# Expert products in chunks of 512 tokens, second product with the relu tiles stationary, state rows as a chunk of their own

## The chip, the cores and the metric

One core of one Trainium2 chip runs the whole program. The metric is the device time of one execution in microseconds (us), lower is better; the times are medians over repeated executions. TensorE multiplies, VectorE (DVE), ScalarE (ACT) and GpSimd (POOL) work on what it leaves in PSUM and SBUF, and SyncE (SP) issues the DMAs.

## What is computed

The reference takes x (4 batches, 8 heads, 512 tokens, 64 wide) and 32 state rows for each batch and head. Attention between tokens and state rows in both directions gives 4 x 544 = 2176 rows of 512 numbers, 512 token rows and 32 state rows for each batch. Then come a dense MLP and eight gated experts:

```python
h = x @ w_in                      # 512 -> 2048
x = (h - np.tanh(h)) @ w_out      # 2048 -> 512
logits = x @ w_gate               # 8 columns
P = np.exp(logits - logits.max())
for _ in range(8):                # Sinkhorn: rows, then columns
    P /= P.sum(1, keepdims=True) + 1e-09
    P /= P.sum(0, keepdims=True) + 1e-09
    P *= N / E
for e in range(E):                # w1: 512 -> 1024, w2: 1024 -> 512
    out += P[:, e:e + 1] * (np.maximum(x @ w1[e], 0.0) @ w2[e])
```

## The kernel before

**Precision.** Most products are made of three: an operand is split into a high part of type fp32r and the rest (w1h and w1l, xh and xl, w2h and w2l, hh and hl), and high x high, high x low and low x high are summed in PSUM. ScalarE makes the high parts and VectorE or GpSimd the low ones. One logical 128-deep product is therefore three matmuls, each with a weight load of its own.

**Stages.** Attention is first (lines 700 to 739 and 961 to 1015 belong to it and to what follows from it). The dense MLP goes over four half blocks of 512 hidden features (`dense`, DH = 4 passes), in each first over the 128 state rows (plain f32 operands, lines 1048 and 1079, 128 columns) and then over four batches of 512 token columns (lines 1059 to 1061 and 1075 to 1077). Its sums stand in `acc`, with features in the partitions and the 2176 rows as columns.

**Experts.** Eight experts follow. Each goes over C = 5 chunks of columns, four of 436 and one of 432 (`N`, `width`, `cols`). A chunk has eight steps f. `up` (lines 1106 to 1108) makes one tile of 128 hidden features: 4 slices k of the input x 3 parts = 12 matmuls, with the w1 tile stationary and the chunk's columns of xh or xl moving. ScalarE then writes the relu, rounded, to hh (line 579), and VectorE the rest to hl (line 782). Two steps later `down` (lines 1120 to 1122) adds this tile's share to four PSUM banks `ypsum`, one for each 128 output features: 12 matmuls, with slices of w2h and w2l stationary and hh or hl moving. There are three hidden tiles, and three PSUM banks for them (NH).

**Gates.** In the first expert's first chunk TensorE makes the logits (lines 1144 and 1145). ScalarE copies them out, SP stores them to DRAM, and loads them back with rows in the partitions (`lg_two`). VectorE and GpSimd run the Sinkhorn steps in chunk 2, and SP stores the gates and loads each expert's row of them, spread to all partitions (`gate`, 218 KB for a chunk). The first expert's outputs are kept in `acc` (line 886) and multiplied by GpSimd later (line 458). For each further chunk VectorE multiplies the four banks by the gate into `ytmp` (line 900), GpSimd adds this to `acc` (line 465), and when all four are done the banks are given free (`s_yfree`). At the end the last two adds are VectorE's (line 944), and SP stores the output by chunks.

**Weights.** During an expert's last chunk ScalarE and VectorE split the next expert's weights (lines 480, 484, 690, 694), and SP loads the tiles behind them.

## Time and profile before

| | |
|---|---|
| median of 3 runs | 1907.54 us (1907.45 to 1908.94) |
| profiled execution, first to last instruction | 1907.4 us |
| TensorE matmul busy | 1888.4 us, 99% of the span |
| TensorE weight load busy | 1744.5 us, 91% |
| VectorE busy | 632.2 us, 33% |
| ScalarE busy | 412.6 us, 22% |
| GpSimd busy | 240.4 us, 13% |
| DMA moved | 64.70 MB |

The profile has no time for the profiled execution beside its span; the median of the runs is 0.1 us above the span. PE is the matmul row of TensorE and PEld its weight loads, which overlap the matmuls. Matmuls are pipelined: the time given for one is from its start to its modelled end, and the next has started by then. So what a matmul costs is the distance from its start to the next one's start, which the text calls its pitch. Lines are those of the kernel printed above.

### The profile page before, as it was taken

Reading aid. Unit: us, or ns where it says so; the run is one execution under the profiler, and the core shown is the slowest. Engines: PE = TensorE matmul, PEld = TensorE weight load, DVE = VectorE, ACT = ScalarE, POOL = GpSimd, SP = SyncE. Lnnn points to the kernel's source line nnn. Section 1 sums busy time; section 2 is a strip of 40 time slices with the busy share of each in tenths; the row PEclk is TensorE's granted clock in tenths of the full one; section 3 lists DMA queues with packets and bytes.
Section 4 is the critical chain, followed back from the end, with each engine's and each line's share of the span. In section 5 each row is a group of like instructions: output and inputs, shape, how many; then the busy total and the mean of one; then the engine's idle time right before and its main releaser. Section 6 shows DMA issues by size and latency. Waiting matters only on the chain.

```text
span 1907.4 us, 24434 instructions
## 1 busy us (share of the span) xinstructions
PE 1888.4 (99%) x9480; PEld 1744.5 (91%) x9480; DVE 632.2 (33%) x1067; ACT 412.6 (22%) x781; POOL 240.4 (13%) x216
## 2 busy tenths in 40 slices
PE   7999999999999999999999999999999999999998
PEld 5887888899999999999999999999999999999998
DVE  6656566533333113311321132113211421142112
ACT  6434444421121112111211121112111211121110
POOL 5100000320312000200110011001100110020001
PEclk9899999999999999999999999999999999999999
DMA  6100101110121002000200020002000200010001
GB/s 226 45 17 27 44 0 50 45 46 1 39 69 34 5 5 77 26 5 5 76 26 5 5 76 26 5 5 76 26 5 5 78 24 5 5 49 24 19 19 37
DMA packets 38700, 64.70 MB, mean 34 GB/s; under 512 B 8896, under 2 KB 16656, under 8 KB 38160
## 3 DMA queue, kind: packets, MB, share of 16 engines
q1 hardware_dynamic: 38672, 64.34, 11.1%
q8 instruction: 16, 0.26, 0.1%
q14 instruction: 12, 0.10, 0.0%
HBM read 59.66 MB, written 4.67 MB: 34 GB/s over the span
## 4 chain that ended last, share of the span: by engine, by line
PE 97%; DVE 1%; ACT 1%; issue 0%; DMA 0%; POOL 0%; DVEq 0%; SPq 0%; ACTq 0%; POOLq 0%
PE bank L1108 13%; PE bank L1106 13%; PE bank L1120 13%; PE bank L1121 13%; PE bank L1107 13%; PE bank L1122 13%; PE bank L1075 3%; PE bank L1077 3%; PE bank L1076 3%; PE bank L1061 1%; PE bank L1060 1%; PE bank L1059 1%; PE bank L1015 1%; PE bank L1048 1%; PE bank L1002 1%
## 5 line engine op out<-in xcount | busy, mean ns | idle before, releaser
L782 DVE SCALAR_TENSOR_TENSOR hl<-bank,hh 128x436 fp32r<-128x436 f32 (+1 forms) x320 | 195.5, 611 | 965.1 <-ACT hh L579 964.9
L1108 PE MATMUL bank<-xh,w1l 128*128 (+2 forms) x1280 | 460.7, 360 | 0.0
L1120 PE MATMUL bank<-hh,w2h 128*128 128x436 f32 (+1 forms) x1280 | 460.6, 360 | 0.0
L1121 PE MATMUL bank<-hl,w2h 128*128 128x436 f32 (+1 forms) x1280 | 460.1, 359 | 0.0
L1106 PE MATMUL bank<-xh,w1h 128*128 (+2 forms) x1280 | 460.1, 359 | 0.0
L1122 PE MATMUL bank<-hh,w2l 128*128 128x436 f32 (+1 forms) x1280 | 459.7, 359 | 0.0
L1107 PE MATMUL bank<-xl,w1h 128*128 (+2 forms) x1280 | 459.1, 359 | 0.0
L579 ACT ACTIVATE hh<-bank 128x436 fp32r<-128x436 f32 (+1 forms) x320 | 170.9, 534 | 1233.0 <-PE bank L1108 1233.0
L465 POOL TENSOR_TENSOR acc<-acc,ytmp 128x436 f32<-128x436 f32 (+1 forms) x138 | 156.7, 1169 | 1164.9 <-DVE ytmp L900 1164.9
L1107 PEld LDWEIGHTS bank<-xl,w1h 128*128 128x128 f32 x1280 | 240.6, 188 | 13.3
L1122 PEld LDWEIGHTS bank<-hh,w2l 128*128 128x128 f32 x1280 | 240.3, 188 | 12.6
L1108 PEld LDWEIGHTS bank<-xh,w1l 128*128 128x128 f32 x1280 | 240.3, 188 | 12.4
L1121 PEld LDWEIGHTS bank<-hl,w2h 128*128 128x128 f32 x1280 | 240.6, 188 | 12.0
L1106 PEld LDWEIGHTS bank<-xh,w1h 128*128 128x128 f32 x1280 | 240.3, 188 | 12.3
L1120 PEld LDWEIGHTS bank<-hh,w2h 128*128 128x128 f32 x1280 | 240.3, 188 | 11.5
L900 DVE TENSOR_TENSOR ytmp<-bank,gate 128x436 f32<-128x436 f32 (+1 forms) x140 | 84.0, 611 | 143.0 <-PE bank L1122 138.2
L1075 PE MATMUL bank<-hh,w2h 128*128 128x512 f32 x256 | 101.8, 398 | 0.0
L1077 PE MATMUL bank<-hh,w2l 128*128 128x512 f32 x256 | 101.4, 396 | 0.0
L1076 PE MATMUL bank<-hl,w2h 128*128 128x512 f32 x256 | 101.4, 396 | 0.0
L777 DVE TENSOR_TENSOR hl<-h_less_tanh,hh 128x512 fp32r<-128x512 f32 x64 | 45.3, 708 | 44.0 <-ACT hh L574 44.0
L1075 PEld LDWEIGHTS bank<-hh,w2h 128*128 128x128 f32 x256 | 48.1, 188 | 12.7 <-DVE acc L795 1.1
L1077 PEld LDWEIGHTS bank<-hh,w2l 128*128 128x128 f32 x256 | 48.2, 188 | 11.7
(101 smaller groups left out, 1166.5 us busy)
## 6 DMA issues: line engine op xcount, KB each, us to landing
st<-w SPq DMA_DIRECT2D x160, 256.0 KB, 2.7
gate<-gate_scratch SPq DMA_DIRECT2D x32, 218.0 KB, 3.0
xT<-xT SPq DMA_DIRECT2D x8, 512.0 KB, 8.2
xn<-xn SPq DMA_DIRECT2D x4, 1024.0 KB, 6.2
out<-acc SPq DMA_DIRECT2D x4, 872.0 KB, 4.2
gate<-gate_scratch SPq DMA_DIRECT2D x8, 216.0 KB, 3.1
out<-acc SPq DMA_DIRECT2D x2, 432.0 KB, 2.8
sT<-sT SPq DMA_DIRECT2D x2, 128.0 KB, 3.8
```

The lines of the kernel that those rows point to most:

```text
L465: nc.gpsimd.tensor_tensor(acc[:, k, cols(c)], acc[:, k, cols(c)], ytmp[:, k % 3, 0:width(c)], ALU.add).then_inc(s_ya, 1)
L579: nc.scalar.activation(hh[:, f % NH, 0:n], hpsum[f % NH][:, 0:n], ACT.Relu).then_inc(s_hh, 1)
L782: v.scalar_tensor_tensor(hl[:, f % NH, 0:n], hpsum[f % NH][:, 0:n], 0.0, hh[:, f % NH, 0:n].bitcast(f32), ALU.max, ALU.subtract).then_inc( ...
L1075: mm(out, w2h[:, s, at], high, start=(s == 0), stop=False)
L1076: mm(out, w2h[:, s, at], hl[:, i % NH, :], start=False, stop=False)
L1077: last = mm(out, w2l[:, s, at], high, start=False, stop=(s == HF - 1))
L1106: mm(out, w1h[:, f, k, :], xh[:, k, cols(c)], start=(k == 0), stop=False)
L1107: mm(out, w1h[:, f, k, :], xl[:, k, cols(c)], start=False, stop=False)
L1108: last = mm(out, w1l[:, f, k, :], xh[:, k, cols(c)], start=False, stop=(k == KT - 1))
L1120: mm(out, w2h[:, f, at], hh[:, f % NH, 0:n], start=(f == 0), stop=False)
L1121: mm(out, w2h[:, f, at], hl[:, f % NH, 0:n], start=False, stop=False)
L1122: last = mm(out, w2l[:, f, at], hh[:, f % NH, 0:n], start=False, stop=(f == F - 1))
```

## The change

- The 2048 token rows and the 128 state rows are kept apart: xh and xl hold the token columns alone (`own_rows`), and new tiles `xsh`, `xsl` the state rows.
- An expert has C = 4 chunks of 512 tokens and, after chunk 1 (`ST_CHUNK`), one of the 128 state rows (`state_up`, `state_down`).
- `down` is turned round: a slice of 128 tokens of hh or hl is stationary, and 512 columns of w2h or w2l move. The outputs have tokens in the partitions (`yacc`, 17 tiles of 128 x 512).
- The gate of a token is then one number for each partition. VectorE multiplies and adds in one instruction (`scalar_tensor_tensor` in `gated`), and gives each bank free alone. GpSimd's adds, the gate tiles, their DMAs and the DRAM scratch go. VectorE copies an expert's gates to a small tile first (`own_gate`), and multiplies the first expert's kept outputs in chunk 3 (`gate_kept`).
- The logits are turned by 17 transposes on TensorE (`turn_logits`) in place of the way through DRAM.
- The output is stored by tokens, the last chunk in four parts of one tile each. Loops over chunks are written out on TensorE and ScalarE.

```diff
-C = 5
-N = 436
+C = B
+ST_TILE = TQ - 1
+ST_CHUNK = 1
+PASSES = C + 1
...
             def up(b, c, f):
...
-                out = hpsum[f % NH][:, 0:width(c)]
+                out = hpsum[f % NH][:]
                 for k in range(KT):
-                    mm(out, w1h[:, f, k, :], xh[:, k, cols(c)], start=(k == 0), stop=False)
-                    mm(out, w1h[:, f, k, :], xl[:, k, cols(c)], start=False, stop=False)
-                    last = mm(out, w1l[:, f, k, :], xh[:, k, cols(c)], start=False, stop=(k == KT - 1))
+                    mm(out, w1h[:, f, k, :], xh[:, k, own_rows(c)], start=(k == 0), stop=False)
+                    mm(out, w1h[:, f, k, :], xl[:, k, own_rows(c)], start=False, stop=False)
+                    last = mm(out, w1l[:, f, k, :], xh[:, k, own_rows(c)], start=False, stop=(k == KT - 1))
                 last.then_inc(s_up, 1)
...
-                if f == 0:
-                    pe.wait_ge(s_yfree, q + 1)
-                for k in range(KT):
-                    out, at = ypsum[k][:, 0:n], slice(k * P, (k + 1) * P)
-                    mm(out, w2h[:, f, at], hh[:, f % NH, 0:n], start=(f == 0), stop=False)
-                    mm(out, w2h[:, f, at], hl[:, f % NH, 0:n], start=False, stop=False)
-                    last = mm(out, w2l[:, f, at], hh[:, f % NH, 0:n], start=False, stop=(f == F - 1))
+                for t in range(ST):
+                    if f == 0:
+                        pe.wait_ge(s_yfree, ST * q + t + 1)
+                    out, at = ypsum[t][:], slice(t * P, (t + 1) * P)
+                    mm(out, hh[:, f % NH, at], w2h[:, f], start=(f == 0), stop=False)
+                    mm(out, hh[:, f % NH, at], w2l[:, f], start=False, stop=False)
+                    last = mm(out, hl[:, f % NH, at], w2h[:, f], start=False, stop=(f == F - 1))
...
+            def state_up(f):
+
+                out = hpsum[f % NH][:, 0:SB]
+                for k in range(KT):
+                    mm(out, w1h[:, f, k, :], xsh[:, k, :], start=(k == 0), stop=False)
+                    mm(out, w1h[:, f, k, :], xsl[:, k, :], start=False, stop=False)
+                    last = mm(out, w1l[:, f, k, :], xsh[:, k, :], start=False, stop=(k == KT - 1))
+                last.then_inc(s_up, 1)
+
+            def state_down(x, f):
+
+                pe.wait_ge(s_hs, DSTEPS + turn(x, C) * F + f + 1)
+                if f == 0 and (not isinstance(x, int) or x):
+                    pe.wait_ge(s_syf, x)
+                mm(stpsum[:], hh[:, f % NH, 0:SB], w2h[:, f], start=(f == 0), stop=False)
+                mm(stpsum[:], hh[:, f % NH, 0:SB], w2l[:, f], start=False, stop=False)
+                last = mm(stpsum[:], hl[:, f % NH, 0:SB], w2h[:, f], start=False, stop=(f == F - 1))
+                if f == F - 1:
+                    last.then_inc(s_sy, 1)
+
+            def state_rows(x):
+
+                for f in range(F):
+                    state_up(f)
+                    if f >= 2:
+                        state_down(x, f - 2)
+                state_down(x, F - 2)
+                state_down(x, F - 1)
...
+            def turn_logits():
+
+                pe.wait_ge(s_lgc, C + 1)
+                for t in range(TQ):
+                    last = nc.tensor.transpose(lgpsum[:, t * 2 * E:(t + 1) * 2 * E], lg_rows[:, t * P:(t + 1) * P],
+                                               ident[0:2 * E, 0:2 * E])
+                last.then_inc(s_lgt, 1)
...
+            def state_input():
+
+                for k in range(KT):
+                    act.wait_ge(s_dsum, KT * (1 + (DH - 1) * DC) + k + 1)
+                    nc.scalar.copy(by_batch(xsh, k), states(acc, k)).then_inc(s_x2h, 1)
...
             def gated(x, c):
...
-                    v.tensor_tensor(ytmp[:, k % 3, 0:n], ypsum[k][:, 0:n], gate[:, c, 0:n], ALU.mult).then_inc(s_ym, 1)
-                dve.wait_ge(s_ym, (x - 1) * (C * KT) + (c + 1) * KT)
-                dve.sem_inc(s_yfree, 1)
+                for t in range(ST):
+                    i = c * ST + t
+                    dve.wait_ge(s_y, ST * (x * C + c) + t + 1)
+                    v.scalar_tensor_tensor(yacc[:, i], ypsum[t][:], gcur[:, i:i + 1], yacc[:, i], ALU.mult,
+                                           ALU.add).then_inc(s_yfree, 1)
...
+            store(ST, 0, ST)
+            store(2 * ST, ST, 2 * ST)
+            sp.wait_ge(s_syf, E)
+            sp.dma_start(out_d[:, ST_TILE:TQ], yacc[:, ST_TILE:TQ]).then_inc(s_out, 16)
+            store(3 * ST, 2 * ST, 3 * ST)
+            for t in range(3 * ST, 4 * ST):
+                store(t + 1, t, t + 1)
```

## Rows read from the trace of the kernel before

**Rows 1.** The page: busy time by engine, and the chain's shares.

```profile
PE 1888.4 (99%) x9480; PEld 1744.5 (91%) x9480; DVE 632.2 (33%) x1067; ACT 412.6 (22%) x781; POOL 240.4 (13%) x216
PE 97%; DVE 1%; ACT 1%; issue 0%; DMA 0%; POOL 0%; DVEq 0%; SPq 0%; ACTq 0%; POOLq 0%
```

**Rows 2.** Busy time by windows, the expert stage and one inner stretch of it.

```profile
core 0: us, PE busy (x) PEld busy (x) DVE busy (x) ACT busy (x) POOL busy (x), PEclk, DMA share, GB/s
377.45:1901.52 1524.07, 1524.07 (x7720) 1449.74 (x7719) 395.88 (x668) 239.05 (x453) 192.03 (x174) 1.00 0.09 28
422.00:612.00 190.00, 190.00 (x965) 180.72 (x964) 65.36 (x145) 29.98 (x57) 27.39 (x30) 1.00 0.12 35
```

**Rows 3.** Timeline of TensorE, the expert stage's first and last matmuls.

```profile
377.22 0.39 PE L1077 MATMUL bank<-hh,w2l 128*128 128x512 f32 x1
377.45 0.36 PE L1106 MATMUL bank<-xh,w1h 128*128 128x436 f32 x1
...
1901.52 0.35 PE L1122 MATMUL bank<-hh,w2l 128*128 128x432 f32 x1
```

**Rows 4.** Timeline of TensorE, a dense stretch of 512 columns, 66 matmuls from first to last.

```profile
80.18 0.40 PE L1075 MATMUL bank<-hh,w2h 128*128 128x512 f32 x1
...
82.98 0.40 PE L1059 MATMUL bank<-xh 128*128 128x512 f32 x1
...
95.57 0.39 PE L1059 MATMUL bank<-xh 128*128 128x512 f32 x1
```

**Rows 5.** The chain: 16 plain f32 passes of 64 columns, then 24 of 128.

```profile
22.27 1.73 PE bank L1002 x16
...
299.40 2.68 PE bank L1048 x24
```

**Rows 6.** Weight loads, groups by line and shape.

```profile
L1106 PEld LDWEIGHTS bank<-xh,w1h 128*128 128x128 f32 x1280 | 240.3, 188 | 12.3
L1002 PEld LDWEIGHTS bank<-a2T,xn 128*128 128x128 f32 x128 | 16.8, 209 | 0.9 <-issue 0.5
L1079 PEld LDWEIGHTS bank<-state_tokens_hidden,st 128*128 128x128 f32 x128 | 16.2, 191 | 0.7
```

**Rows 7.** VectorE and ScalarE groups by line and shape.

```profile
L795 DVE TENSOR_TENSOR acc<-bank,acc 128x512 f32<-128x512 f32 x64 | 40.8, 684 | 11.4 <-PE bank L1077 11.3
L769 DVE TENSOR_TENSOR state_tokens_hidden<-bank,tanh_h 128x128 f32<-128x128 f32 x16 | 4.6, 286 | 3.4 <-ACT tanh_h L564 3.4
L564 ACT ACTIVATE tanh_h<-bank 128x128 f32<-128x128 f32 x16 | 4.4, 278 | 26.3 <-PE bank L1048 24.5 <-DVE state_tokens_hidden L769 1.0
L694 DVE TENSOR_TENSOR w2l<-st,w2h 128x512 fp32r<-128x512 f32 x63 | 57.2, 925 | 0.9
L777 DVE TENSOR_TENSOR hl<-h_less_tanh,hh 128x512 fp32r<-128x512 f32 x64 | 45.3, 708 | 44.0 <-ACT hh L574 44.0
```

**Rows 8.** Timeline of VectorE at the end.

```profile
1900.27 2.44 DVE L900 TENSOR_TENSOR ytmp<-bank,gate 128x432 f32<-128x432 f32 x4 [4.15 <-PE bank L1122]
1902.86 1.25 DVE L944 TENSOR_TENSOR acc<-acc,ytmp 128x432 f32<-128x432 f32 x2
```

**Rows 9.** DMA issues: size of one, median us from issue to landing.

```profile
st<-w SPq DMA_DIRECT2D x160, 256.0 KB, 2.7
gate<-gate_scratch SPq DMA_DIRECT2D x32, 218.0 KB, 3.0
out<-acc SPq DMA_DIRECT2D x2, 432.0 KB, 2.8
```

More of the change, by code:

```diff
@@ L112, in build @@
         amax = sb("amax", [P, 1])
-        assert place[0] <= gates + C * N * 4
+        hiddens = place[0]
+        hh = sb("hh", [P, NH, S], f32r)
+        hl = sb("hl", [P, NH, S], f32r)
+        xsh = sb("state_rows_hi", [P, KT, SB], f32r)
+        xsl = sb("state_rows_lo", [P, KT, SB], f32r)
+        scratch = place[0]
+        end = place[0]
+        place[0] = scratch
+        wg_raw = sb("wg_raw", [P, KT, E])
+        wg = sb("wg", [P, KT, P], f32r)
+        lg_rows = sb("lg_rows", [2 * E, T])
+        lg_two = sb("lg_two", [P, TQ, 2 * E])
+        end = max(end, place[0])
         place[0] = after_w2l - (F - HF) * DM * 4
@@ L146, in build @@
         r1 = sb("r1", [P, 2, 4 * ST])
-        end = max(end, place[0])
+        assert place[0] <= scratch
         assert end <= nc.sbuf_usable_end, (end, nc.sbuf_usable_end)
@@ L156, in build @@
         lgpsum = bank[7]
+        stpsum = bank[7]
         mpsum = bank[7]
@@ L529, in m_hi @@
                     rows = slice(pair_first(b, kp), pair_first(b, kp) + 2 * NS)
-                    nc.scalar.copy(xh[rows, 2 + kp // 2, batch(b)], bank[rows, :]).then_inc(s_mh, 1)
+                    nc.scalar.copy(xh[rows, 2 + kp // 2, own_rows(b)], bank[rows, :]).then_inc(s_mh, 1)
             for i in range(2):
@@ L598, in dense @@
                         w1_hi(DENSE, HF + s)
+                    if last and s == 2 and j == 1:
+                        state_input()
                     if last and s == 2 and j >= 2:
@@ L614, in logits_exp, with chunk @@
                     nc.scalar.activation(pr[:], pr[:], ACT.Exp, bias=amax[:, 0:1]).then_inc(s_exp, 1)
-            def chunk(b, c, split, extra=None):
-                q = (b - DENSE) * C + c
+            def chunk(b, c, extra=None):
+                x, q = b - DENSE, (b - DENSE) * C + c
+                split = c == C - 1 and extra is not last_chunk
                 for f in range(F):
-                    hidden_expert(q, f, width(c))
+                    hidden_expert(turn(x, c), f)
                     if extra is not None:
@@ L865, in sinkhorn, with chunk @@
                 rows(f)
-            def chunk(b, c, split, extra=None):
-                q = (b - DENSE) * C + c
+            def chunk(b, c, extra=None):
+                x, q = b - DENSE, (b - DENSE) * C + c
+                split = c == C - 1 and extra is not last_chunk
                 for f in range(F):
-                    hidden_expert(q, f, width(c))
+                    hidden_expert(turn(x, c), f)
                     if extra is not None:
@@ new lines, in _, with gate_some @@
+            chunk(DENSE, 0, gating)
+            dve.wait_ge(s_x2s, (C + 1) * KT)
+            keep(0)
+            chunk(DENSE, 1, logits_max)
+            keep(1)
+            state_rows(0)
+            keep_states()
+            chunk(DENSE, 2, sinkhorn)
+            keep(2)
+            columns(SINKHORN - 1)
+            def gate_some(f):
+                for t in range(2 * f, min(2 * f + 2, 3 * ST)):
+                    gate_kept(t)
+                if f == F - 1:
+                    gate_kept(ST_TILE)
@@ L930, in _, with expert @@
+            chunk(DENSE, 3, gate_some)
+            gated_first(3)
             last_w2(DENSE)
-            def expert(b, split):
+            def expert(b, end=False):
+                x = b - DENSE
+                own_gate(x)
                 for c in range(C):
-                    chunk(b, c, split and c == C - 1)
-                    gated(b - DENSE, c)
-                if split:
-                    last_w2(b)
-            with dve.Fori(DENSE + 1, NB - 1) as b:
-                expert(b, True)
@@ L941, in _ @@
-            expert(NB - 1, False)
-            for k in range(KT // 2, KT):
-                v.tensor_tensor(acc[:, k, cols(C - 1)], acc[:, k, cols(C - 1)], ytmp[:, k % 3, 0:width(C - 1)],
-                                ALU.add).then_inc(s_last, 1)
+                    chunk(b, c, last_chunk if end else None)
+                    gated(x, c)
+                    if c == ST_CHUNK:
+                        state_rows(x)
+                        gated_states(x)
+                if not end:
+                    last_w2(b)
@@ L1153, in _ @@
             dense(DH - 1, last=True)
-            pe.wait_ge(s_x2s, KT)
+            pe.wait_ge(s_x2s, 2 * KT)
             chunk(DENSE, 0, gating=True)
-            with pe.Fori(1, C - 1) as c:
+            pe.wait_ge(s_lgr, 1)
+            for c in range(1, C):
                 chunk(DENSE, c)
-            chunk(DENSE, C - 1)
             with pe.Fori(DENSE + 1, NB) as b:
-                with pe.Fori(0, C - 1) as c:
+                for c in range(C):
                     chunk(b, c)
-                chunk(b, C - 1)
 def kernel(**inputs):
```

304 lines of the change are left out of this document (131 added, 173 removed).

## The prediction

> **What bounds the kernel now.** I read the busy times and the chain's shares first [rows 1]: TensorE's matmuls are busy for 99% of the span, and 97% of the chain that ended last is TensorE. No other engine passes 33%. Busy time alone says little where matmuls overlap, so I next asked the windows for the expert stage from its first matmul to its last [rows 2], whose ends come from TensorE's timeline [rows 3]: 1524.07 us, 7720 matmuls, granted clock 1.00 (2.4 GHz). TensorE is busy through every one of these microseconds. 7720 is 8 experts x 5 chunks x 8 steps x 24 = 7680, and 40 for the logits. The mean pitch is 1524.07 / 7720 = 197.4 ns. The inner stretch gives 190.00 / 965 = 196.9 ns, so there is no place where the stage stalls. The chunks' mean width is 2176 / 5 = 435.2 columns, so a column costs 197.4 / 435.2 = 0.4536 ns.
>
> So the expert stage is a gapless stream of matmuls, and what VectorE, GpSimd and SP do beside it costs nothing as long as it stays beside it. The change is worth what it does to the number of matmuls and their pitch, plus what it does behind the last matmul.
>
> **Matmuls removed and added.** The columns that move are the same. Up: 12 matmuls over 2176 columns in each step, before and after. Down, before: 12 over 2176 columns = 26112. Down, after: 12 of 512 columns for each of four chunks and 3 for the states, 51 x 512 = 26112. What changes is how they are cut:
> - 512 columns: up 12 x 4 x 64 = 3072, down 3072, state down 3 x 64 = 192, logits 4 x 8 = 32. Together 6368.
> - 128 columns, each with a weight load of 128 columns: state up 12 x 64 = 768, logits 8. Together 776.
> - 17 transposes of logits, 16 columns each.
>
> Together 7161 in place of 7720.
>
> **Price at 512 columns.** The dense stage has the same kind (three-part products, a load for each, the same clock). From 80.18 to 95.57 us there are 66 of them, 12 down and 6 up in turn, without a gap [rows 4]: 15.39 / 66 = 233.2 ns. The per-column price of the expert stage gives 0.4536 x 512 = 232.3 ns. I take 232.5. Turning the down product round puts a hidden tile in the load and w2 in the stream; both sides of the dense products (1059 to 1061 have xh on both sides, 1075 to 1077 hidden tiles moving) run at nearly the same pitch, 2.80 us for 12 from 80.18 to 82.98 (233.3), so I give the turning itself nothing. Low end: if the excess over the bare column time, 197.4 - 435.2 / 2.4 = 16.1 ns, is one fixed price for each matmul, 512 columns cost 213.3 + 16.1 = 229.4. High end 234.
>
> 6368 x 232.5 = 1480.6 us.
>
> **Price at 128 columns.** No row before shows an fp32r matmul under 432 columns, and on this one unknown most of the result hangs. Lowest bound: the column price alone, 0.4536 x 128 = 58 ns; with the fixed 16.1 it is 53.3 + 16.1 = 69.4. Nearest rows in size: the plain f32 passes, of which two make one product. 24 of 128 columns take 2.68 us, 111.7 ns each; 16 of 64 columns take 1.73 us, 108 ns each [rows 5]. Half the columns save almost nothing, so at these sizes something other than the columns sets the pitch, and each of these passes has its load of 128 columns. The loads of fp32r take 188 ns by the record and those of plain f32 191 [rows 6], start to end with the latency in it, so I expect the same floor for both kinds. At 436 or 512 columns the load is hidden behind the stream; behind 128 columns it isn't. Highest bound: a whole product at 128 columns costs no less in this mode than in plain f32, two passes, 2 x 111.7 = 223.4 ns. I take 111.7, since the rows say "load", and loads of both kinds look alike.
>
> 776 x 111.7 = 86.7 us. 17 transposes at 111.7 (loads again) = 1.9 us.
>
> The Trainium skill (TensorE: Matmul & The Clock Gate, section LDWEIGHTS) puts a load at the columns of the stationary operand over 1.2 GHz, 106.7 ns for 128. The trace agrees with it at the small sizes, 108 and 111.7 [rows 5]; by 106.7 the two terms above would be 4 us less. The same page's section on the back-to-back gap gives N / 2.4 + 2.5 ns for a matmul alone, 184 at 436 columns against the measured 197.4, and some 81 ns for pairs of load and matmul at 128 columns; by 81 the state rows would cost 24 us less than I count.
>
> **Sum of the stage.** 1480.6 + 86.7 + 1.9 = 1569.2 us against 1524.07: +45.1 us. Put as a balance: the 6368 at 232.5 and the transposes leave (1524.1 - 1482.5) / 776 = 53.6 ns for each 128-column matmul before the change loses, and the columns alone take 53.3.
>
> **What lies beside it, and costs nothing.** VectorE in a chunk of 48 x 4 = 192 matmuls, 44.6 us: eight hl tiles at about 0.7 us (L777) and four gated tiles at 0.68 (L795, [rows 7], the same operands of one bank and one of SBUF) are 8.4 us; with sixteen splits at up to 0.93 in the last chunk 23 us. `gate_kept` adds 13 x 0.7 us in one chunk. All of that is cover of over 20 us a chunk. If it were gone the 4 x 0.68 us would stand in front of the next chunk's `down`. It has three `up` tiles, 36 x 0.2325 = 8.4 us, before it needs a bank, and the banks come free one at a time. GpSimd's multiplies and adds go, and free time that nobody waits for. The gate DMAs (218 KB each, [rows 9]) go from SP's queue; behind them there stood only the weight loads, whose consumers have a whole chunk.
>
> State rows: a step is 12 x 0.112 + 3 x 0.2325 = 2.0 us of TensorE against one relu of 128 columns, 0.28 us, and one rest, 0.29 us [rows 7]. At the end `state_down(7)` needs its hidden tile 1.4 us after the last `state_up`, and relu and rest take about 0.65 with their hand-overs. At 58 or 70 ns a step is 1.4 us or more, still covered. At the start VectorE has the fourth bank to gate (0.7 us) before the first state tile; TensorE has three `state_up`, 4.0 us. `turn_logits` waits for a copy whose logits TensorE made a step (5.6 us) earlier. `state_input` is four small ScalarE copies (about 0.28 each) in the last dense pass, over a step of some 4.9 us. The Sinkhorn steps get 5.6 us for each f instead of 4.7. `own_gate` is one small copy on VectorE behind the last bank. I price all these waits at 0 to 3 us together and take 0.
>
> **The end.** Before: last matmul starts at 1901.52 and ends near 1901.9, VectorE's last multiply ends at 1902.71, its two adds at 1904.11 [rows 8], then 3.3 us to the end of the span for issue, landing (2.8, [rows 9]) and waiting. After: one fused instruction of 0.68 us from about 1901.95, then a DMA of 256 KB, 2.7 in place of 2.8 (st<-w). End to end 0.68 + 3.2 instead of 5.5: -1.5 us.
>
> **Total** 1907.4 + 45.1 - 1.5 = 1951.0 us, 2.3% slower. This is against the profiled span, which is 0.1 us under the median; I predict 1951. Its own range: 512 columns at 229.4 to 234 is -20 to +10 us, waits 0 to +3, so 1931 to 1964.
>
> **Rivals.**
> - *Narrow matmuls are charged as full f32.* If fp32r at 128 columns loses its single pass and costs what two plain passes do, 223.4 ns, the 776 cost 173.4 us: 1951.0 + 86.7 = 2037.7. For it: no narrow fp32r matmul is in the trace, and the kernel's narrow products (L1048, L1079) are of the plain kind. Against it: nothing but the similar loads. Chance 0.27.
> - *The load hides, the fixed price stays.* 776 x 69.4 = 53.9, so 1480.6 + 53.9 + 1.9 = 1536.4, +12.3 - 1.5: 1918.2. The 108 ns at 64 columns speaks against it, unless plain f32 loads are slower than they look. Chance 0.08.
> - *Columns alone.* All matmuls cost 0.4536 ns a column. The columns are equal, so only transposes and the end are left: 1907.4 + 1.9 - 1.5 = 1907.8, no change. Chance 0.06.
> - *Faster: fewer matmuls, each with a fixed price.* With 229.4 at 512 and 69.4 at 128 columns: 1460.8 + 53.9 + 1.9 = 1516.6, -7.5 - 1.5: 1898.4. It decides once 512 columns cost 229.4 and a 128-column matmul stays under (1524.1 + 1.5 - 1460.8 - 1.9) / 776 = 81 ns. For it: 559 matmuls less, and 16.1 ns of excess on each. Against it: 233.2 measured at 512 columns and 108 at 64. Chance 0.09.
>
> The skill's isolated gap is the page's form of the last two: by it the stage would come out the same, since 6368 at 215.8 and 776 at 55.8 equal 7720 at about 184. The trace has 197.4 and 233.2 in those places.
>
> **How the numbers follow.** The forecast has 0.50, the rivals 0.27, 0.08, 0.06 and 0.09. What a measurement of this kernel can tell from no change is about 0.2%, 3.8 us. Slower: 0.50 + 0.27 + 0.08 = 0.85. Same 0.06, faster 0.09. The range must hold the forecast's own 1931 to 1964 and the first rival's 2038, since leaving out the latter alone would lose 0.27; it reaches down to 1918 for the second. 1915 to 2042.
>
> **What would show it.** In the profile after, the stream of 512-column matmuls should have a pitch of 232 to 233 ns in up and in turned down alike. The twelve matmuls of `state_up` should follow each other at 112 ns: 8 experts x 96 x 112 ns is the 86 us. Their pitch is the number that decides between all cases (58, 69, 112, 223). TensorE should have no gap over 0.3 us at the edges of chunks and of state rows. The expert stage should begin near 377.5 us, and about 4.0 us should lie between the last matmul's end and the end of the span. The forecast is wrong if the state pitch is far from 112, if 512 columns cost another price with the hidden tiles stationary (6368 matmuls: each ns is 6.4 us), or if the written-out loops or the state rows' hand-overs make TensorE stop.

## The result and the profile after

The changed kernel takes 1943.46 us (median, 1942.33 to 1944.25), the kernel before 1908.24 us beside it (1907.45 to 1909.29). The ratio is 1.0182, with a 95% interval of 1.017 to 1.0194: 35 us slower.

The profiled execution of after spans 1940.2 us, and its own time is 1942.33, so 2.1 us lie around the span. For the kernel before that distance is 1.8 us wherever a span and a time of the same execution are known (1908.86 against 1907.1, 1907.53 against 1905.7): its profiled span of 1907.4 belongs to an execution of about 1909.2 us, and the 0.1 us that stands ahead of the prediction compares different executions. So the spans differ by 32.8 us and the medians by 35.2. Busy time by engine, the chain's shares, and the queue that brings instructions, from the page of after (they answer to [rows 1]):

```profile
PE 1920.1 (99%) x8921; PEld 1576.4 (81%) x8921; DVE 626.7 (32%) x1061; ACT 413.6 (21%) x782; POOL 59.8 (3%) x58
q8 instruction: 77, 1.26, 0.3%
PE 97%; issue 1%; DVE 1%; ACT 1%; POOL 0%; DVEq 0%; ACTq 0%; POOLq 0%
```

TensorE has 559 matmuls less and is busy 32 us longer. GpSimd fell from 240 to 60 us, and nobody waited for that. The windows of the expert stage, whose ends come from TensorE's timeline (they answer to [rows 2, 3]):

```profile
378.94:1936.52 1557.58, 1557.58 (x7161) 1284.28 (x7160) 390.28 (x664) 238.40 (x450) 9.20 (x13) 1.00 0.07 22
```

```profile
378.70 0.40 PE L1081 MATMUL bank<-hh,w2l 128*128 128x512 f32 x1
378.94 0.40 PE L1110 MATMUL bank<-xh,w1h 128*128 128x512 f32 x1
...
1936.52 0.39 PE L1126 MATMUL bank<-w2h,hl 128*128 128x512 f32 x1
```

The stage went from 1524.07 to 1557.58 us, +33.5, at the same clock and still busy from end to end. The rest of the difference lies at the two ends of the span: the stage starts 1.49 us later (378.94 against 377.45), and between the last matmul's start and the end of the span there are 3.7 us where there were 5.9, -2.2. Sum: 33.5 + 1.5 - 2.2 = 32.8 us, the difference of the spans (1940.2 - 1907.4).

Three kinds of matmul are to be seen in TensorE's timeline. Inside one step, twelve up matmuls (the last three are shown), then twelve down (the first is shown), and the next step's first up:

```profile
600.75 0.39 PE L1110 MATMUL bank<-xh,w1h 128*128 128x512 f32 x1
600.97 0.39 PE L1111 MATMUL bank<-xl,w1h 128*128 128x512 f32 x1
601.20 0.39 PE L1112 MATMUL bank<-xh,w1l 128*128 128x512 f32 x1
601.43 0.39 PE L1124 MATMUL bank<-w2h,hh 128*128 128x512 f32 x1
...
604.24 0.40 PE L1110 MATMUL bank<-xh,w1h 128*128 128x512 f32 x1
```

The ups shown follow each other at about 0.227 us; the twelve downs take 604.24 - 601.43 = 2.81, 234 ns each. And at the start of the state rows, 36 `state_up` matmuls:

```profile
477.05 0.40 PE L1126 MATMUL bank<-w2h,hl 128*128 128x512 f32 x1
477.28 0.22 PE L1134 MATMUL bank<-state_rows_hi,w1h 128*128 128x128 f32 x1
477.34 0.27 PE L1135 MATMUL bank<-state_rows_lo,w1h 128*128 128x128 f32 x1
477.45 0.27 PE L1136 MATMUL bank<-state_rows_hi,w1l 128*128 128x128 f32 x1
...
481.13 0.28 PE L1136 MATMUL bank<-state_rows_hi,w1l 128*128 128x128 f32 x1
481.25 0.45 PE L1144 MATMUL bank<-w2h,hh 128*128 128x512 f32 x1
```

From 477.34 to 481.25 there are 35 pitches, 111.7 ns each. The first narrow one has a pitch of only 0.06: its load ran behind the wide matmul before it. The bill comes on the other side, where a wide one (L1144) follows on narrow ones.

Summing all distances between starts over the stage gives the whole account:

| kind | number | predicted each, sum | measured mean, sum |
|---|---|---|---|
| up, 512 columns | 3072 | 232.5 ns, 714.2 us | 227.5 ns, 699.0 us |
| down turned, 512 | 3072 | 232.5, 714.2 | 234.1, 719.1 |
| state down, 512 | 192 | 232.5, 44.6 | 244.5, 46.9 |
| state up, 128 | 768 | 111.7, 85.8 | 108.2, 83.1 |
| logits, 512 and 128 | 40 | 8.3 us | 8.3 us |
| transposes | 17 | 111.7, 1.9 | 68.6, 1.2 |
| together | 7161 | 1569.2 us | 1557.6 us |

What lies beside the stream, from the groups by line and shape, VectorE's timeline at the end, and the DMA issues (they answer to [rows 6 to 9]):

```profile
L1134 PEld LDWEIGHTS bank<-state_rows_hi,w1h 128*128 128x128 f32 x256 | 49.0, 191 | 2.1
L747 DVE SCALAR_TENSOR_TENSOR hl<-bank,hh 128x512 fp32r<-128x512 f32 x256 | 177.2, 692 | 909.1 <-ACT hh L532 909.1
L881 DVE SCALAR_TENSOR_TENSOR yacc<-bank,gate_now,yacc 128x512 f32<-128x512 f32 x112 | 80.1, 751 | 132.8 <-PE bank L1126 132.8
```

```profile
1934.85 2.85 DVE L881 SCALAR_TENSOR_TENSOR yacc<-bank,gate_now,yacc 128x512 f32<-128x512 f32 x4 [5.00 <-PE bank L1126]
```

```profile
out<-yacc SPq DMA_DIRECT2D x5, 256.0 KB, 2.0
```

The fused gate and add takes 751 ns, and VectorE waits for TensorE before it, not the other way round. The last of the four ends at 1937.70, and 2.5 us later the span ends.

### The profile page after: what moved, and what is told of

Same layout as the page of the kernel before. It is cut to its first block, busy times and chain, and to the rows that moved or that the text cites. A ratio compares the mean times of both kernels' runs of the same rounds, so it can differ in the third digit from the quotient of the medians.

```text
span 1940.2 us, 22124 instructions
## 1 busy us (share of the span) xinstructions
PE 1920.1 (99%) x8921; PEld 1576.4 (81%) x8921; DVE 626.7 (32%) x1061; ACT 413.6 (21%) x782; POOL 59.8 (3%) x58
## 3 DMA queue, kind: packets, MB, share of 16 engines
q8 instruction: 77, 1.26, 0.3%
## 4 chain that ended last, share of the span: by engine, by line
PE 97%; issue 1%; DVE 1%; ACT 1%; POOL 0%; DVEq 0%; ACTq 0%; POOLq 0%
PE bank L1124 12%; PE bank L1126 12%; PE bank L1125 12%; PE bank L1110 12%; PE bank L1112 12%; PE bank L1111 12%; PE bank L1079 3%; PE bank L1081 3%; PE bank L1080 3%; PE bank L1136 1%; PE bank L1135 1%; PE bank L1063 1%; PE bank L1064 1%; PE bank L1065 1%; PE bank L1134 1%; PE bank L1019 1%
## 5 line engine op out<-in xcount | busy, mean ns | idle before, releaser
L747 DVE SCALAR_TENSOR_TENSOR hl<-bank,hh 128x512 fp32r<-128x512 f32 (+1 forms) x320 | 195.8, 612 | 1002.2 <-ACT hh L532 1002.2
L1124 PE MATMUL bank<-w2h,hh 128*128 128x512 f32 x1024 | 406.9, 397 | 0.0
L1126 PE MATMUL bank<-w2h,hl 128*128 128x512 f32 x1024 | 405.5, 396 | 0.0
L1125 PE MATMUL bank<-w2l,hh 128*128 128x512 f32 x1024 | 404.9, 395 | 0.0
L1110 PE MATMUL bank<-xh,w1h 128*128 128x512 f32 x1024 | 399.8, 390 | 0.0
L1111 PE MATMUL bank<-xl,w1h 128*128 128x512 f32 x1024 | 399.0, 390 | 0.0
L1112 PE MATMUL bank<-xh,w1l 128*128 128x512 f32 x1024 | 398.9, 390 | 0.0
L1126 PEld LDWEIGHTS bank<-w2h,hl 128*128 128x128 f32 x1024 | 193.1, 189 | 47.8
L1125 PEld LDWEIGHTS bank<-w2l,hh 128*128 128x128 f32 x1024 | 192.5, 188 | 46.5
L1124 PEld LDWEIGHTS bank<-w2h,hh 128*128 128x128 f32 x1024 | 192.2, 188 | 44.2
```

The source lines that it names most:

```text
L747: v.scalar_tensor_tensor(hl[:, f % NH, 0:n], hpsum[f % NH][:, 0:n], 0.0, hh[:, f % NH, 0:n].bitcast(f32), ALU.max, ALU.subtract).then_inc( ...
L1110: mm(out, w1h[:, f, k, :], xh[:, k, own_rows(c)], start=(k == 0), stop=False)
L1111: mm(out, w1h[:, f, k, :], xl[:, k, own_rows(c)], start=False, stop=False)
L1112: last = mm(out, w1l[:, f, k, :], xh[:, k, own_rows(c)], start=False, stop=(k == KT - 1))
L1124: mm(out, hh[:, f % NH, at], w2h[:, f], start=(f == 0), stop=False)
L1125: mm(out, hh[:, f % NH, at], w2l[:, f], start=False, stop=False)
```

## The experiments

Times of timed kernels are medians, with a ratio to the kernel before on the same chip. "One run" is one profiled execution, read for its pitches and not for its time.

### Narrow matmuls of other sizes (one run)

The sizes of `state_up` go by its steps f: two as in the change, two with 64 moving columns, two with 256 (token columns), two with 64 columns of w1 stationary. Its output isn't the reference's.

```diff
             def state_up(f):
...
+                    elif f < 4:
+                        out = bank_f[:, 0:64]
+                        mm(out, w1h[:, f, k, :], xsh[:, k, 0:64], start=first, stop=False)
...
+                    elif f < 6:
+                        out = bank_f[:, 0:256]
+                        mm(out, w1h[:, f, k, :], xh[:, k, 0:256], start=first, stop=False)
...
+                    else:
+                        out = bank_f[0:64, 0:SB]
+                        mm(out, w1h[:, f, k, 0:64], xsh[:, k, :], start=first, stop=False)
```

> The changed kernel, with the state rows' first product cut four ways by step, so its numbers are not the reference's: steps 0 and 1 as they are (128 columns move, 128 are stationary), 2 and 3 with 64 moving, 4 and 5 with 256 moving, 6 and 7 with 128 moving and only 64 stationary. Theory (the weight load sets the pitch of a narrow matmul): 112 ns, then 108 to 112 at 64 moving (no gain), about 120 at 256 moving (256 / 2.4 = 107 and the 14 of the 512-column stream), and 59 to 70 with 64 stationary columns. Rival (a narrow fp32r matmul runs at two cycles a column, 128 x 2 / 2.4 = 107 ns): about 58 at 64 moving, 213 or more at 256 moving unless that counts as wide, and 112 unchanged with 64 stationary.

TensorE's timeline of this kernel: 64 columns moving, 256 moving, and 128 moving behind a stationary tile of 64 columns:

```profile
484.25 0.28 PE L1144 MATMUL bank<-state_rows_hi,w1l 128*128 128x64 f32 x1
484.36 0.28 PE L1142 MATMUL bank<-state_rows_hi,w1h 128*128 128x64 f32 x1
...
486.05 0.28 PE L1149 MATMUL bank<-xh,w1l 128*128 128x256 f32 x1
486.16 0.28 PE L1147 MATMUL bank<-xh,w1h 128*128 128x256 f32 x1
486.28 0.28 PE L1148 MATMUL bank<-xl,w1h 128*128 128x256 f32 x1
...
490.23 0.22 PE L1152 MATMUL bank<-state_rows_hi,w1h 128*64 128x128 f32 x1
490.29 0.22 PE L1153 MATMUL bank<-state_rows_lo,w1h 128*64 128x128 f32 x1
```

Medians over the eight experts, by line: 111 to 112 ns for 128 moving columns, 111 to 112 for 64, 117.5 to 120 for 256, and 59 to 60 for 128 columns behind a load of 64. So at 128 moving columns and fewer neither the columns nor a fixed price sets the pitch, the load does, and it goes with the columns of the stationary tile. The loads' own records agree: 192 ns for 128 stationary columns and 135 for 64. The Trainium skill (TensorE: Matmul & The Clock Gate, section LDWEIGHTS) has a load at its columns over 1.2 GHz, 106.7 ns for 128 and 53.3 for 64; the runs show 112 and 60, a few ns more.

### Narrow matmuls mixed in among wide ones (4 runs)

All the computation stays; in chunk 1 each down matmul is followed by one narrow matmul that is extra work, into the bank of the state rows before these use it.

```diff
                     mm(out, hh[:, f % NH, at], w2h[:, f], start=(f == 0), stop=False)
+                    if c == ST_CHUNK:
+                        mm(stpsum[:, 0:SB], w1h[:, f, t, :], xsh[:, t, :], start=True, stop=True)
```

(and the same behind the other two parts, with xsl and w1l)

> The changed kernel with 96 more narrow matmuls for each expert, 768 in all (copies of the state rows' first product whose result is overwritten), one behind each wide matmul of chunk 1's second product. Theory (each narrow matmul exposes the load of the next one, wherever it stands): +112 ns each, +86 us, 2029 us. Rival (behind a wide matmul two loads fit, so a narrow one costs its columns alone, 58 to 60 ns): +45 us, 1988 us; then mixing the state rows into the token chunks would give back some 40 us.

2027.66 us, ratio 1.0623 (1.0607 to 1.0639). Over the changed kernel that is 84.2 us for 768 extra matmuls, 110 ns each. TensorE's timeline:

```profile
1258.62 0.39 PE L1124 MATMUL bank<-w2h,hh 128*128 128x512 f32 x1
1258.85 0.22 PE L1126 MATMUL bank<-state_rows_hi,w1h 128*128 128x128 f32 x1
1258.91 0.44 PE L1127 MATMUL bank<-w2l,hh 128*128 128x512 f32 x1
1259.19 0.22 PE L1129 MATMUL bank<-state_rows_lo,w1h 128*128 128x128 f32 x1
1259.25 0.45 PE L1130 MATMUL bank<-w2h,hl 128*128 128x512 f32 x1
```

A narrow one has a pitch of 0.06 and the wide one behind it 0.28, together 340 ns, where a wide one alone has 234. As I read it, the narrow one hides its own load behind the wide one, but the next load has only the narrow one's 128 columns to hide behind. So placing narrow matmuls between wide ones gives nothing back. What helps is not to have them.

### No chunk of its own for the state rows (11 runs)

The whole computation, with the turned down product. The 17 tiles of 128 rows, state rows as the last, go in five chunks of 3, 3, 4, 4 and 3 tiles, so up moves 384 or 512 columns and never 128.

```diff
-ST_CHUNK = 1
-PASSES = C + 1
+CHUNKS = ((0, 3), (3, 3), (6, 4), (10, 4), (14, 3))
+NC = len(CHUNKS)
...
-        xh = sb("xh", [P, KT, B * S], f32r)
+        xh = sb("xh", [P, KT, T], f32r)
```

> The whole computation. The second product stays turned, the gates by token, the logits transposed and the loops written out, but the 128 state rows are no chunk of their own: 17 tiles of 128 rows in five chunks of 3, 3, 4, 4 and 3 tiles (384 or 512 columns). Theory (the separate narrow chunk is the loss): first product 768 x (3 x 174 + 2 x 227.5) ns = 750 us, second 3264 x 234.2 = 764.4, logits and transposes 10: 1524 us, the stage of the kernel before; with the shorter end 1905 to 1911 us in all, no change from before and 33 to 37 us under the changed kernel. Rival (the turned product, the written-out loops and their instruction fetches are part of the loss): 1920 to 1940 us.

1911.98 us (1909.98 to 1912.55), ratio 1.0014 (1.0005 to 1.0023): 31.5 us faster than the changed kernel with the same products, the same turned down and the same fused gate. The window of its expert stage:

```profile
380.12:1906.58 1526.46, 1524.99 (x7162) 1311.69 (x7160) 389.85 (x661) 238.41 (x450) 9.56 (x13) 1.00 0.07 22
```

31.1 us less than 1557.58. The up matmuls of 384 columns have a pitch of 174.5 ns, those of 512 227.4; down is at 233.8, and five stops of 0.25 to 0.56 us where the expert loop starts again come on top. The time is 1 us above the 1905 to 1911 that was expected; these stops are 2.3 us together. For the state rows, up now costs 3 x 174.5 - 2 x 227.4 = 69 ns in the place where the changed kernel pays 108 for a matmul of its own. The down matmuls sum to 765.5 us here and to 766.0 in the changed kernel, so the gain is all in up. So the separate narrow chunk is the loss, shown by taking it away and keeping the rest of the change.

### Down not turned (4 runs)

The changed kernel with w2 slices stationary and the hidden tiles moving again, for the tokens and the state rows. Its output is not that of the reference, since the gates are still applied by tokens; the matmuls are of the right number and size, 768 of them now 128 wide in `state_down`.

```diff
-                    mm(out, hh[:, f % NH, at], w2h[:, f], start=(f == 0), stop=False)
+                    mm(out, w2h[:, f, at], hh[:, f % NH, :], start=(f == 0), stop=False)
...
-                mm(stpsum[:], hh[:, f % NH, 0:SB], w2h[:, f], start=(f == 0), stop=False)
+                for k in range(KT):
+                    out, at = stpsum[:, k * SB:(k + 1) * SB], slice(k * P, (k + 1) * P)
+                    mm(out, w2h[:, f, at], hh[:, f % NH, 0:SB], start=True, stop=False)
```

> The changed kernel with only the second product turned back (w2 slices stationary, hidden tiles moving), for tokens and states. The outputs then stand by feature and are gated as if they stood by token, and each state product is closed alone, so the numbers are not the reference's. Theory (turning costs the tokens nothing and spares the states narrow matmuls): token matmuls stay at 234 ns; the states have 12 matmuls of 128 columns a step, 768 x 112 ns = 86 us, in place of 192 of 512 columns, 47 us: +39 us, 1982 us. Rival (turning is what makes 512 columns cost 234 instead of 227.5): tokens fall to 227.5, -20 us, and the whole comes to 1962.

1990.42 us (1988.85 to 1990.91), ratio 1.0427 (1.0412 to 1.0443), 47 us slower than the changed kernel. `state_down` costs 768 x 111.7 = 85.8 us in place of 46.9: +38.9. The tokens' down is at 234 either way, so turning costs nothing, and spares the state rows 39 us. The missing 8 us were not expected. The stage starts 1.4 us later. `state_up` rose by 2.1 us: its first matmul now follows a narrow one, behind which its load can't hide (the mean of its first line is 109.8 ns and was 101.6). And the up matmuls rose by 4.8 us (703.8 against 699.0), though they are the same. One step's twelve, the first of each half and the down behind them:

```profile
605.79 0.40 PE L1110 MATMUL bank<-xh,w1h 128*128 128x512 f32 x1
...
607.18 0.40 PE L1110 MATMUL bank<-xh,w1h 128*128 128x512 f32 x1
...
608.55 0.40 PE L1124 MATMUL bank<-hh,w2h 128*128 128x512 f32 x1
```

Taken over all such steps, the first six have a mean pitch of 231.5 ns with hidden tiles moving in the down product before them, and only from the ninth on is it 227. In the changed kernel, with hidden tiles stationary there, the first two are at 232.9 and 230.6, and the third and later ones at 226.6 to 228.1. Why a matmul is slowed by those before it isn't shown.

### Why down is at 234 and up at 227: three tries

*Other operands (one run).* The output isn't the reference's: in chunk 1 all four token tiles add into the last bank (but for the last step), in chunk 2 slices of xh and xl are stationary in place of hh and hl, in chunk 3 xh and xl move in place of w2h and w2l; chunk 0 is as it was.

```diff
+                    if c == 2:
+                        mm(out, xh[:, t, at], w2h[:, f], start=(f == 0), stop=False)
...
+                    if c == 3:
+                        mm(out, hh[:, f % NH, at], xh[:, t, 0:S], start=(f == 0), stop=False)
```

> The changed kernel; a 512-column matmul takes 227.5 ns in the first product and 234 in the second, and this asks why. The second product differs by chunk, so its numbers are not the reference's: chunk 0 as it is, chunk 1 with all tiles of steps 0 to 6 in one PSUM bank, chunk 2 with slices of xh and xl stationary in place of the hidden tiles, chunk 3 with xh and xl moving in place of w2. If the change of bank costs the 6.5 ns, chunk 1 falls to 227 to 228 and the others stay at 234. If the freshly written stationary tile does, chunk 2 falls alone. If the moving tile does, chunk 3 falls alone. If it is none of them, all stay at 234. Whole time within 5 us of the changed kernel's 1943 in every case.

TensorE's timeline, every third down matmul, chunk 0 as it was (L1150), chunk 2 with xh stationary (L1137), chunk 3 with xh moving (L1144):

```profile
1169.82 0.39 PE L1150 MATMUL bank<-w2h,hh 128*128 128x512 f32 x1
1170.52 0.40 PE L1150 MATMUL bank<-w2h,hh 128*128 128x512 f32 x1
...
1274.71 0.39 PE L1137 MATMUL bank<-w2h,xh 128*128 128x512 f32 x1
1275.39 0.39 PE L1137 MATMUL bank<-w2h,xh 128*128 128x512 f32 x1
...
1318.23 0.39 PE L1144 MATMUL bank<-xh,hh 128*128 128x512 f32 x1
1318.93 0.40 PE L1144 MATMUL bank<-xh,hh 128*128 128x512 f32 x1
```

0.70 for three with hh stationary, whatever moves; 0.68 with xh stationary. Means: 234.3, 226.7 and 234.1 ns, and 234.1 with all tiles in one bank. What is slow is the hidden tile as an operand. The up matmuls of chunk 2 are at 226.5 to 226.8 from the first on, so it is the hidden tiles too that slow the first ups elsewhere. I first took the fast chunk for the one with the single bank. The expectations of the experiments on banks, and what that of 448 columns says of one bank, rest on that misreading, and their results put it right.

*Banks.* Two experiments. In the first the mixed chunks' down takes two steps at a time, so that six matmuls in a row go to one bank (5 runs). In the second, one run whose output isn't the reference's, the four tiles of chunks 0 to 3, but for the last step, add into bank 0 alone, bank 1 alone, banks 2 and 3, and banks 0 and 3.

```diff
-            def down(b, c, f):
+            def down(b, c, fs):
...
+                    for f in fs:
+                        mm(out, hh[:, f % NH, at], w2h[:, f], start=(f == 0), stop=False)
```

> The whole computation: the kernel of five mixed chunks, with the second product done for two steps at a time, so that six matmuls in a row go to one PSUM bank in place of three (steps 0 to 5; the last two singly). Theory (a change of bank disturbs the next few matmuls): the pitch of these 2448 matmuls falls from 234 to some 229.5, -11 us, 1901 us, under the kernel before. Rival (it is not the change but which bank or what stands in it): 234 stays, 1912 us.

```diff
+                to = ((0, 0, 0, 0), (1, 1, 1, 1), (2, 3, 2, 3), (0, 3, 0, 3))[c]
...
+                    out = ypsum[t if own else to[t]][:]
```

> The changed kernel; all of the second product's tiles went to bank 3 in one chunk of an earlier run and took 227 ns in place of 234, yet six in a row for each bank took 234 as well. Here steps 0 to 6 write, by chunk: 0 all to bank 0, 1 all to bank 1, 2 in turn to banks 2 and 3, 3 in turn to banks 0 and 3; so the numbers are not the reference's. Theory (it is the number of the bank, 0 to 2 being slower than 3 to 6): chunk 0 and 1 take 234, chunk 2 lies between, chunk 3 too. Rival (any change of bank within a step starts the slow pattern, and it lasts): chunks 0 and 1 take 227, chunks 2 and 3 take 234.

The first: 1916.8 us, ratio 1.0044 (1.0031 to 1.0058), the down pitch stayed at 234.0, and six times TensorE stood for 0.7 to 1.2 us at the restart of its loop, once in an expert; 4.8 us slower than without. The second: 234.1 to 234.3 ns in all four chunks. A third is below: output and hidden banks exchanged, no pitch moved. The bank has no part in it.

*Where the tile begins (11 runs).* From the kernel's own allocation, w1, w2, xh and xl begin within their partition on multiples of 64 bytes that all leave the same remainder by 256. hh and hl begin 32 bytes past a multiple of 64, before and after; their remainder by 256 is 160 bytes past that of w1 before, and 96 after. In the two kernels with a packed gate tile (below) hh and hl happen to have w1's remainder; there the dense stage's matmuls with hh or hl moving are at 227.2 ns and not 233.9, and the expert stage starts at 371.0 us and not 377.45. The dense stage's instructions are the same, and its hidden tiles as freshly written, in both. So I placed hh and hl, in the best kernel of the turned kind, on a multiple of 128. The whole computation.

```diff
+        place[0] = (place[0] + 127) // 128 * 128
         hiddens = place[0]
         hh = sb("hh", [P, NH, S], f32r)
```

> The whole computation: the kernel of e10_banks_swapped (five mixed chunks, early start) with one edit, the tiles of the down product's hidden activations hh and hl, and the small tiles behind them, start on a multiple of 128 bytes within their partition; in e10 they start 32 bytes past a multiple of 64. Theory (a matmul of 512 columns whose operand starts off such a multiple is paced at 234 ns and not at 227, whichever of its two operands it is): the down product's pitch falls from 234.2 to about 227 ns, 3264 x 7 = 23 us, and the dense stage, whose down product moves hh, ends 6 us earlier (the expert stage begins at about 370 and not at 375.7); the total is 1908.9 - 23 - 6 = about 1880 us, range 1876 to 1885. Rival (the tile was slow because it is freshly written by VectorE and ScalarE, and xh and xl were fast because they were written long before, or are not being written by another engine at the time): no pitch moves, 234 stays, the total stays within 1907 to 1911. If only the dense stage moves, the alignment works for the moving operand alone: about 1903.

1906.8 us (1905.27 to 1908.62), ratio 0.999 (0.9981 to 0.9999), against 1908.92 without the edit. The 3264 down matmuls fell only from 765.3 to 760.4 us in all (234.5 to 233.0 ns), and up rose from 751.4 to 755.2, though its operands stand where they stood; the dense stage's down went from 234.0 to 232.7, and the expert stage starts at 374.8 and not 375.7. The theory as I put it (such a multiple is enough) fell. The rival (the tile is slow because it is freshly written) said that no pitch would move; a move of 1.5 ns out of 7 speaks only weakly against it, but the dense stage of the two kernels with a packed gate tile does plainly, for their tiles are as fresh and at 227. hh now began on a multiple of 128, but not with the remainder of w1 and xh by 256; that placement wasn't tried in the turned kernel, and what the rule is stays open.

### The start (8 runs)

The kernel with two steps for each bank, with one wait moved: TensorE waits for the identity only ahead of the first transpose.

```diff
-            pe.wait_ge(s_ident, 1)
             scores_T(0)
+            pe.wait_ge(s_ident, 1)
             scores_N(0)
```

> The whole computation: as the run with two steps for each bank, and TensorE's wait for the identity stands behind the first scores instead of ahead of them. In the changed kernel and all made from it GpSimd's second instruction starts at 9 us instead of 1.4, and TensorE's first matmul with it at 9.6 instead of 6.6. Theory (that late instruction is all that delays the start): -1.5 to -3 us against the run with two steps for each bank. Rival (the transposes then wait for it just as long): within 0.5 us.

1914.12 us, ratio 1.0029 (1.0018 to 1.0039), 2.7 us less than without, and the stage starts at 377.47 and not 380.08.

GpSimd and TensorE in the changed kernel show what was waited for:

```profile
0.73 0.20 POOL L379 MEMSET ident<- 128x128 f32 x1 [0.29 <-POOLq L1243]
9.23 0.28 POOL L381 TENSOR_SCALAR_AFFINE_SELECT ident<-ident 128x128 f32<-128x128 f32 x1 [8.30 <-issue]
...
9.61 1.94 PE L965 MATMUL bank<-xT,sT 128*64 128x512 f32 x3 [9.61 <-POOL ident L381]
```

In before the same instruction starts at 1.43 us and TensorE at 6.58, when its input has landed. GpSimd stands for 8.30 us on nothing that the profile shows.

### Mixed chunks, early start, banks exchanged (11 runs)

```diff
-        ypsum = bank[0:4]
-        hpsum = bank[4:4 + NH]
+        ypsum = bank[NH:NH + 4]
+        hpsum = bank[0:NH]
```

> The whole computation: the five mixed chunks with the early start, and the banks swapped, hidden products in banks 0 to 2 and outputs in 3 to 6. If the number of the bank sets the price, the second product falls to 227 (-23 us) and the first rises to 234 at 512 columns (+10 us at most): 1895 to 1900 us. If the change of bank does, nothing moves: 1909 us, which is the run of five mixed chunks (1912) less the 2.7 us of the early start.

1908.92 us (1907.35 to 1909.63), ratio 1.0 (0.9991 to 1.001). Pitches as they were; the stage runs from 375.68 to 1901.89 us. The turned kernel is now level with the one before.

### The kernel before with other widths (5 runs each)

If every matmul carried a fixed price, chunks of 448 columns (four, and one of 384) would be no dearer in sum than those of 436. Both kernels below are whole computations. The gate tile is packed without gaps to make room, which moves hh as said.

```diff
-N = 436
+N = 448
...
-        gate = sb("gate", [P, C, N])
+        gate = sb("gate", [P, T])
```

> The whole computation: the kernel before with the chunk width alone changed from 436 to 448 (four of 448 and one of 384 columns; the gate tile is packed to fit). The stream's price over the bare columns is 13.5 ns at 384 and 512 columns in one bank, but 16 at 436. Theory (436 is an awkward width, and the excess is one fixed price): first product at 200.2 and 173.7 ns; if the second product, with a bank change every three, gets the same, 1536 x (4 x 200.2 + 173.7) = 1497 us in place of 1515.5: -18 us, 1890; if only the first product gains, -9 us, 1900. Rival (the columns alone count): no change, 1909.

1921.38 us, ratio 1.0064 (1.005 to 1.0078). TensorE's timeline, from the end of the dense stage into the experts:

```profile
370.28 0.39 PE L1075 MATMUL bank<-hh,w2h 128*128 128x512 f32 x1
370.51 0.39 PE L1076 MATMUL bank<-hl,w2h 128*128 128x512 f32 x1
370.73 0.39 PE L1077 MATMUL bank<-hh,w2l 128*128 128x512 f32 x1
370.96 0.36 PE L1106 MATMUL bank<-xh,w1h 128*128 128x448 f32 x1
...
1153.73 0.37 PE L1120 MATMUL bank<-hh,w2h 128*128 128x448 f32 x1
1153.94 0.37 PE L1121 MATMUL bank<-hl,w2h 128*128 128x448 f32 x1
```

448 columns cost 206.6 ns, 0.461 a column, against 0.4536 at 436 and 0.443 at 512. The theory fell: a fixed part and a part by columns through the 173.4 ns of its 384 columns and 227 at 512 would give 200. At the same time the stage starts 6.5 us earlier.

The other way, four chunks of 432 and one of 448:

```diff
-N = 436
+N = 432
+NL = 448
```

> The whole computation: the kernel before with chunk widths of 432, 432, 432, 432 and 448 columns in place of 436 and 432. Prices read so far in this kernel: 432 columns 194 ns in the last chunk of the kernel before, 436 197.9, 448 206.6. Theory (each width has its own price, wherever it stands): 1536 x (4 x 194.5 + 206.6) = 1512 us in place of 1515.5, -3 us, 1905 us. Rival (432 was cheap because of where that chunk stands, beside ScalarE's and VectorE's splits): 1536 x (4 x 197 + 206.6) = 1528, +12 us, 1921 us.

1901.56 us (1899.88 to 1902.8), ratio 0.9961 (0.9947 to 0.9975), faster than both kernels. It was expected at 1905 us, with 194.5 ns for 432 columns and 206.6 for 448 wherever they stand. The window of its expert stage:

```profile
371.05:1893.86 1522.81, 1522.81 (x7720) 1453.72 (x7719) 395.87 (x668) 239.39 (x453) 192.28 (x174) 1.00 0.09 28
```

1.3 us come from the widths, 6.4 from the dense stage that ends earlier. The prices behind that sum were both off: 432 columns cost 195.9 ns, and 448, which are the last chunk here, 202.7 and not the 206.6 of the kernel above, in which the up matmuls of the first expert's first chunk are at 203.1 too. So a width doesn't have one price wherever it stands, and why isn't known.

## Why the prediction came out as it did

The forecast case held. Its 1951.0 us is a span (it starts from the 1907.4 of before), and the measured span is 1940.2, 10.8 less: 11.6 in the stage and 0.7 at the end, against 1.5 at the start. That the median, 1943.46, lies nearer is luck, since 2.1 us lie around the span and the prediction counted 0.1.

One more row of before's TensorE belongs beside [rows 4], for the second step below: the first down matmul behind the six up ones that start at 82.98.

```profile
84.38 0.40 PE L1075 MATMUL bank<-hh,w2h 128*128 128x512 f32 x1
```

Step by step:

- **Price at 128 columns**, on which most hung: 111.7 ns foreseen, 111.7 in the steady stream, 108.2 as a mean, because the first of twelve hides its load wherever it follows a wide matmul (48 of 64 times). The rows could have said it more firmly: the 108 ns for 64 columns [rows 5] is 1.73 us over 16 matmuls, and in the trace of before the first of them has a pitch of 58 ns and the fifteen behind it 112, as at 128 columns. The reason was right too: halving the moving columns leaves 112, halving the stationary ones gives 60. The rivals at 223, 69 and 58 ns fell with that.
- **Price at 512 columns**, the term that was mis-sized: "I take 232.5" for both products. Down measured 234.1, +4.8 us, and up 227.5: 699.0 us in place of 714.2, -15.3 us, more than all of what the forecast was too high. It also lies under the 229.4 of the low end. The step that failed is the carrying over of the dense stage's pitch [rows 4]. It has both kinds in one stretch, twelve matmuls with hidden tiles and six without, but reading each kind alone wouldn't have helped: a group of six without, from 82.98 [rows 4] to the 84.38 above, take 1.40 us, 233 ns each, and over the whole stretch they have 231.7 ns and the twelve 233.8. The runs show that the hidden tile as an operand, where it lies in these kernels, costs 7 ns, moving or stationary, and that it slows the matmuls behind it: six and more of them where it moves, as in the dense stage and in down not turned, two where it is stationary. So all the dense up matmuls stand in its reach, and ten of the changed kernel's twelve don't.
- **Turning the product costs nothing**: right, 234 either way, and it gives back 4.8 us in the up matmuls behind it, which was not foreseen. That it spares the state rows three quarters of their down matmuls was in the counts, and measured 39 us.
- **State down**: 244.5 in place of 232.5, +2.3 us. The first wide matmul behind narrow ones pays its own load in part (the 340 ns for a pair, in the mixed-in experiment). This was not foreseen, nor the about equal gain on the other side, -2.7 us.
- **Transposes**: 68.6 and not 111.7 ns, -0.7 us.
- **Waits "0 to 3 us together and take 0"**: right. In the stage two pitches beside the transposes exceed 0.3 us (0.32 and 0.34), none at the edges of chunks or of state rows.
- **The end**: -1.5 foreseen, -2.2 measured. The fused instruction takes 0.75 us and not 0.68, and 256 KB landed in 2.0 and not 2.7.
- **The start**: nothing foreseen, +1.5 measured, GpSimd's late identity. That it comes from fetching instructions was only argued, from the instruction queue's 77 packets and 1.26 MB, against 16 and 0.26 in before; what the early-start run shows is that TensorE's early wait for the identity cost 2.6 us in the kernel with two steps for each bank.

Sum of the stage: 45.1 - 15.3 + 4.8 + 2.3 - 2.7 - 0.7 = 33.5, as measured.

The balance of the prediction can now be put right. With 1472 us for everything in the stage but the 776 narrow matmuls at measured prices (699.0 + 3264 x 0.2342 + 32 x 0.233 + 1.2), they may cost (1524.1 - 1472.0) / 776 = 67 ns each before the change loses. They cost 108 on average.

## What to carry to other kernels

Ask of each matmul whether its moving columns cover the next load: with a full stationary tile 64 and 128 columns don't here (112 ns either way), and 256 just do (119 ns). A remainder of 128 rows is cheaper spread over the other chunks (three of 384 columns) than in a chunk of its own, which cost 31 us. A product can be turned round at no cost in the stream, and then the turn pays where it makes narrow matmuls into wide ones. When a price is carried over from another stretch, ask what stands before each matmul there, and not only what its own shape is: 5 ns on 3072 up matmuls were 15 us.

## What the runs showed that was not expected

- The pitch isn't straight in the columns: 174.5 ns at 384, 195.9 at 432, 202.7 to 206.6 at 448, 227 or 234 at 512, that is 0.454, 0.453, 0.452 to 0.461 and 0.443 or 0.457 a column.
- The dense stage's down matmuls are at 227 or 234 ns by where the hidden tile lies in SBUF, and neighbours whose operands didn't move change with it (6.5 us in all). Bank numbers change nothing.
- Where a long loop body starts again, once in an expert, TensorE stood for 0.1 to 0.6 us in the kernels with mixed chunks, for 0.7 to 1.2 us in the two of them with two steps for each bank, and not at all in the changed one. The traces show no engine that it waited for.
